# Routing of an attention and experts kernel: early places ahead of the last logits, row and column by an integer mask, ScalarE squares the decay and marks four tiles

## The reference

```python
# 1. decaying linear attention: B=2, H=8, S=768, D=64, blocks of 64
intra = (q_b @ k_b^T * Dmask) @ v_b                  # Dmask = lam ** (i - j) for i >= j
inter = (q_b * lam ** (i + 1)) @ kv_state
out_b = intra + inter
kv_state = lam ** 64 * kv_state + (k_b * lam ** (63 - j))^T @ v_b
# 2. mixture of experts: N=1536 tokens, 512 features, E=8 experts of width 1024, the best one only
logits = x @ w_gate; e = argmax(logits); gate = softmax(logits)[e]
y = gate * (relu(x @ w1[e]) @ w2[e])
# 3. dense layer, width 2048
h = y @ w_in; out = (h - tanh(h)) @ w_out
```

## Time and profile before

| | us |
|---|---|
| median of 3 runs | 526.89 |
| lowest, highest | 526.42, 528.42 |
| profiled execution, its own time | 527.13 |
| its span, first to last instruction | 525.4 |
| TensorE busy in the span | 507.6 |
| VectorE, ScalarE, GpSimd busy | 361.3, 258.2, 318.1 |
| mean granted TensorE clock | 0.993 |

### The profile page before, as it was taken

The page is one execution under the profiler, slowest core; times in us unless marked ns, Lnnn a source line. Parts: engine busy times, 40 slices in busy tenths (PEclk is TensorE's granted clock), DMA queues, the critical chain, the costliest instruction groups (busy, mean ns, idle before and its releaser), DMA issues.

```text
span 525.4 us, 10760 instructions
## 1 busy us (share of the span) xinstructions
PE 507.6 (97%) x3809; PEld 450.0 (86%) x3810; DVE 361.3 (69%) x546; ACT 258.2 (49%) x474; POOL 318.1 (61%) x261
## 2 busy tenths in 40 slices
PE   5999989999999999999999999999999999999994
PEld 4878879999999999999888888888888888888883
DVE  7555546654545545454599999979987766997781
ACT  1333417666666666656454545544444444544441
POOL 4857057655545545555499898958765454865543
PEclk9999899999999999999999999999999999999998
DMA  8879348778777777774620000001100000100002
GB/s 310 305 250 361 146 120 284 240 198 233 211 222 236 197 232 230 203 238 120 218 106 1 1 2 0 1 0 40 41 1 1 0 1 3 58 21 2 1 0 80
DMA packets 32409, 64.54 MB, mean 123 GB/s; under 512 B 3696, under 2 KB 7792, under 8 KB 32368
## 3 DMA queue, kind: packets, MB, share of 16 engines
q1 hardware_dynamic: 30448, 57.71, 34.8%
q0 software_dynamic: 1920, 6.29, 3.5%
HBM read 57.69 MB, written 6.29 MB: 122 GB/s over the span
## 4 chain that ended last, share of the span: by engine, by line
PE 92%; DMA 3%; POOL 1%; DVE 1%; issue 1%; ACT 1%; SPq 0%; ACTq 0%; POOLq 0%; DVEq 0%
PE bank L325 27%; PE bank L327 27%; PE bank L326 27%; PE bank L1177 3%; PE bank L1151 2%; DMA x_sorted<-token_rows,tokid 2%; PE bank L1197 1%; DMA qk_in<-in_qk_t_dram 1%; PE bank L1163 1%; PE bank L1188 1%; PE bank L1204 1%; POOL x_sorted L634 1%; POOL w_l L626 0%; PE bank L1362 0%; PE bank L1267 0%
## 5 line engine op out<-in xcount | busy, mean ns | idle before, releaser
L626 POOL TENSOR_TENSOR w_l<-wst,w_h 128x512 fp32r<-128x512 f32 x64 | 87.0, 1359 | 78.0 <-ACT w_h L737 77.9
L675 POOL TENSOR_SCALAR big<-h_sq 128x512 uint8<-128x512 f32 x48 | 80.4, 1674 | 36.0 <-ACT h_sq L823 35.8
L689 POOL TENSOR_TENSOR g_l<-g,g_h 128x512 fp32r<-128x512 f32 x46 | 61.2, 1331 | 43.0 <-ACT g_h L833 43.0
L325 PE MATMUL bank<-wo_h,g_h 128*128 128x512 f32 x192 | 75.5, 393 | 0.1
L327 PE MATMUL bank<-wo_l,g_h 128*128 128x512 f32 x192 | 75.1, 391 | 0.0
L326 PE MATMUL bank<-wo_h,g_l 128*128 128x512 f32 x192 | 74.6, 389 | 0.0
L327 PE MATMUL bank<-x_l,win_h 128*128 128x512 f32 x188 | 74.3, 395 | 0.0
L325 PE MATMUL bank<-x_h,win_h 128*128 128x512 f32 x188 | 73.9, 393 | 0.0
L326 PE MATMUL bank<-x_h,win_l 128*128 128x512 f32 x188 | 73.7, 392 | 0.0
L325 PE MATMUL bank<-xs_h,w_h 128*128 (+1 forms) x256 | 70.8, 276 | 0.8 <-DVE xs_l L1045 0.8
L325 PE MATMUL bank<-h_h,w_h 128*128 128x232 f32 x256 | 70.3, 275 | 0.0
(11 more groups left out here) (152 smaller groups left out, 1102.8 us busy)
## 6 DMA issues: line engine op xcount, KB each, us to landing
wst<-in_w_dram SPq DMA_DIRECT2D x128, 256.0 KB, 3.0
qk_in<-in_qk_t_dram SPq DMA_DIRECT2D x12, 512.0 KB, 6.4
kv_in<-in_kv_dram SPq DMA_DIRECT2D x12, 512.0 KB, 5.6
win<-in_w_in_dram SPq DMA_DIRECT2D x8, 512.0 KB, 4.6
wo<-in_w_out_dram SPq DMA_DIRECT2D x8, 512.0 KB, 8.4
token_rows<-x_sb SPq DMA_DIRECT2D x12, 256.0 KB, 5.9
x_sorted<-token_rows,tokid POOLq DMA_INDIRECT x12, 4.2
out_dram<-rows,tokid POOLq DMA_INDIRECT x12, 3.0
```

Source lines behind the costliest of these rows:

```text
L325: pe.matmul(dst, lh, rh, start=start, stop=False, skip_group_check=True)
L626: pool.tensor_tensor(w2_l[:, j % STG], wst2[:, j % STG], w2_h[:, j % 2].bitcast(F32), ALU.subtract).then_inc(w2l_ready, 1)
L675: pool.tensor_scalar(big[:, f % 2], h_sq[:, f % 2], T * T, None, ALU.is_ge).then_inc(big_ready, 1)
L689: pool.tensor_tensor(g_l[:, f % 2], g[:, f % 2], g_h[:, f % 2].bitcast(F32), ALU.subtract).then_inc(gl_ready, 1)
```

## The change

- SyncE loads both forms of the decay factors in one DMA. ScalarE squares them (six squares) and makes `q_pow` by doubling, with four multiplies a step; VectorE's squares and GpSimd's doubling go.
- GpSimd's half of the mask waits until VectorE has finished the first half with its diagonal (`mask_ready` 1).
- TensorE runs the first four heads of tile 0 on v ahead of the scores of tile 1, and waits for `w_gate` at the first gate logits only.
- Behind the loop: places of tiles 0 to 7, then the last gate logits, then both last transposes, then the places of tiles 8 to 11. Before: transposes of tile 10, last logits, transposes of tile 11, early places, three keep-awakes, late places.
- Column and row of a place come from an integer mask (place and -128, and the rest); the comparison with 13 limits and its reduction go.
- ScalarE marks the rows of tiles 8 to 11, as relu(1 - (row - n)^2), between its last x_sb and its first expert weights; VectorE marks tiles 0 to 7.
- GpSimd runs one small indirect DMA of 16 rows (from w_out, into a buffer that is written later) once all tiles have their outputs, and waits for it, ahead of its wait for the token numbers.

The diff without declarations of buffers and semaphores, the DMA of the factors and some unchanged lines:

```diff
@@ -563,6 +566,7 @@
 
             pool.wait_ge(far_step, 6)
             pool.wait_ge(near_step, 10)
+            pool.wait_ge(mask_ready, 1)
             mask_blocks(pool, head_halves[1]).then_inc(late_blocks_ready, 1)
 
...
@@ -588,21 +592,13 @@
 
             pool.wait_ge(mask_ready, 2)
             k_decayed(0)
-            pool.wait_ge(lam_pair_in, 16)
-            pool.tensor_copy(q_pow[:, :, 0:1], lam_pair_sb[:].rearrange("p (a n) -> p a n", n=1)).then_inc(qpow_step, 1)
-            n = 1
-            while n < P:
-                pool.wait_ge(qpow_step, n.bit_length())
-                pool.tensor_tensor(q_pow[:, :, n:2 * n], q_pow[:, :, 0:n],
-                                   q_pow[:, :, n - 1:n].to_broadcast([P, PAIRS, n]), ALU.mult).then_inc(qpow_step, 1)
-                n *= 2
             k_decayed(1)
-            pool.wait_ge(qpow_step, POW_STEPS)
 
             pool.memset(ones[:], 1.0).then_inc(consts, 1)
             pool.wait_ge(consts, 2)
             pool.affine_select(out=tri[:], in_=ones[:], compare_op=ALU.is_gt, fill=0.0, base=0,
                                pattern=[[1, P]], channel_multiplier=-1).then_inc(consts, 1)
+            pool.wait_ge(qpow_step, POW_STEPS)
             for t in range(B, NT):
                 q_decayed(t)
                 if t < NT - B:
...
+            pool.memset(some_row[:], 0).then_inc(consts, 1)
+            pool.wait_ge(consts, 10)
+            pool.wait_ge(o_done, NT)
+            pool.indirect_dma_start(
+                out=x_sorted[0:REHEARSED, NT - 1, :], out_offset=None, in_=w_out,
+                in_offset=bass.IndirectOffsetOnAxis(ap=some_row[0:REHEARSED, :], axis=0)).then_inc(rehearsed, 16)
+            pool.wait_ge(rehearsed, 16)
             for u in range(UN):
                 pool.wait_ge(x_stored[u], 16 * (NT // UN))
...
         def _(act):
 
+            act.wait_ge(lam_in, 16)
+            for i in range(1, 7):
+                ge(act, lam_step, i - 1)
+                act.activation(lam_pow[:, i], lam_sb[:, 0:H] if i == 1 else lam_pow[:, i - 1],
+                               ACT.Square).then_inc(lam_step, 1)
+
+            act.copy(q_pow[:, :, 0:1], lam_sb[:, H:].rearrange("p (a n) -> p a n", n=1)).then_inc(qpow_step, 1)
+            n = 1
+            while n < P:
+                act.wait_ge(qpow_step, n.bit_length())
+                for p in range(PAIRS):
+                    i = act.mul(q_pow[:, p, n:2 * n], q_pow[:, p, 0:n], q_pow[:, p, n - 1:n])
+                i.then_inc(qpow_step, 1)
+                n *= 2
+
             def x_t(t):
...
+
+            act.wait_ge(consts, 9)
+            act.wait_ge(row_ready, 1)
+            for t in range(BY_DVE, NT):
+                act.activation(off_row[:, t], row_no[:], ACT.Square, bias=row[:, t:t + 1],
+                               scale=-1.0).then_inc(off_row_ready, 1)
+            for t in range(BY_DVE, NT):
+                act.wait_ge(off_row_ready, t - BY_DVE + 1)
+                act.activation(in_row[:, t], off_row[:, t], ACT.Relu, bias=1.0, scale=-1.0).then_inc(late_rows_ready, 1)
 
             w1_high(0, 0)
...
@@ -872,13 +899,7 @@
             dve.tensor_copy(diagonal[:], own_block[:]).then_inc(seeds, 1)
 
             dve.wait_ge(lam_in, 16)
-            dve.tensor_tensor(lam_pow[:, 1], lam_sb[:], lam_sb[:], ALU.mult).then_inc(lam_step, 1)
             dve.wait_ge(seeds, 5)
-
-            def square(i):
-
-                dve.wait_ge(lam_step, i - 1)
-                dve.tensor_tensor(lam_pow[:, i], lam_pow[:, i - 1], lam_pow[:, i - 1], ALU.mult).then_inc(lam_step, 1)
 
...
@@ -887,11 +908,9 @@
                 if i:
                     dve.wait_ge(lam_step, i)
                     dve.wait_ge(near_step, 2 * i)
-                lam_n = lam_sb[:] if i == 0 else lam_pow[:, i]
+                lam_n = lam_sb[:, 0:H] if i == 0 else lam_pow[:, i]
                 dve.tensor_tensor(near_part[:, :, n:end], near[:, :, 0:end - n], every(lam_n, end - n),
                                   ALU.mult).then_inc(near_step, 1)
-                if i + 2 < 7:
-                    square(i + 2)
                 dve.wait_ge(near_step, 2 * i + 1)
                 dve.tensor_tensor(near[:, :, n:end], near[:, :, n:end], near_part[:, :, n:end], ALU.add).then_inc(near_step, 1)
...
@@ -989,16 +1008,15 @@
             dve.wait_ge(places_done, 1)
             dve.tensor_tensor(place_of[:], psPos, one_hot[:], ALU.mult).then_inc(route_step, 1)
             dve.wait_ge(route_step, 3)
-            dve.tensor_reduce(place_f[:], place_of[:], AX.X, ALU.add).then_inc(route_step, 1)
+            with nc.allow_low_precision(reason="whole numbers below 4096"):
+                dve.tensor_reduce(place_i[:], place_of[:], AX.X, ALU.add).then_inc(route_step, 1)
             dve.wait_ge(route_step, 4)
-            dve.tensor_tensor(past_col[:], col0[:, :].rearrange("p (a e) -> p a e", a=1).to_broadcast([P, NT, NT + 1]),
-                              place_f[:, :].rearrange("p (t a) -> p t a", a=1).to_broadcast([P, NT, NT + 1]),
-                              ALU.is_le).then_inc(route_step, 1)
+            dve.tensor_scalar(col[:], place_i[:], -P, None, ALU.bitwise_and).then_inc(route_step, 1)
             dve.wait_ge(route_step, 5)
-            dve.tensor_reduce(col[:], past_col[:, :, 1:], AX.X, ALU.add).then_inc(route_step, 1)
-            dve.wait_ge(route_step, 6)
-            dve.scalar_tensor_tensor(row[:], col[:], -float(P), place_f[:], ALU.mult, ALU.add).then_inc(row_ready, 1)
-            dve.tensor_tensor(in_col[:], past_col[:, :, 0:NT], past_col[:, :, 1:], ALU.subtract).then_inc(route_step, 1)
+            dve.tensor_tensor(row[:], place_i[:], col[:], ALU.subtract).then_inc(row_ready, 1)
+            dve.tensor_tensor(in_col[:], col0[:, :].rearrange("p (a e) -> p a e", a=1).to_broadcast([P, NT, NT]),
+                              col[:, :].rearrange("p (t a) -> p t a", a=1).to_broadcast([P, NT, NT]),
+                              ALU.is_equal).then_inc(route_step, 1)
             dve.wait_ge(row_ready, 1)
...
@@ -1010,10 +1028,10 @@
                     ALU.is_equal).then_inc(rows_ready, t1 - t0)
 
             mark_rows(0, 4)
-            dve.wait_ge(route_step, 7)
+            dve.wait_ge(route_step, 6)
             dve.tensor_tensor(ids[:, :, 0], in_col[:], tile_no[:], ALU.mult)
             dve.tensor_scalar(ids[:, :, 1], in_col[:], token_no[:, 0:1], None, ALU.mult).then_inc(ids_ready, 1)
-            for t in range(4, NT, 4):
+            for t in range(4, BY_DVE, 4):
                 mark_rows(t, t + 4)
...
@@ -1172,6 +1190,7 @@
                 for h in range(H):
                     a, p = divmod(h, PAIRS)
                     if t == 0 and h == PAIRS:
+                        scores(1)
                         pe.wait_ge(sm_ready, 1)
                     g, half = divmod(p, 2)
...
@@ -1206,9 +1227,7 @@
                 j.then_inc(logits_done, 1)
 
             scores(0)
-            scores(1)
             pe.wait_ge(ident_ready, 1)
-            pe.wait_ge(w_gate_in, 16)
             for t in range(NT):
                 if t > 1:
...
@@ -1221,12 +1240,6 @@
                     gate_logits(t - 1)
                 if t < NT - B:
                     state_step(t)
-            x_transposes(NT - 2)
-            gate_logits(NT - 1)
-            x_transposes(NT - 1)
-            pe.wait_ge(consts, 3)
...
@@ -1241,8 +1254,11 @@
                                   start=False, stop=True, skip_group_check=True)
                 return i
 
+            pe.wait_ge(consts, 3)
             places(0, EARLY, 0)
-            keep_awake(pe, 3)
+            gate_logits(NT - 1)
+            x_transposes(NT - 2)
+            x_transposes(NT - 1)
             places(EARLY, NT, 1).then_inc(places_done, 1)
             for t in range(NT):
                 i = pe.matmul(psCnt, ones[:], one_hot_b[:, t], start=t == 0, stop=t == NT - 1)
...
@@ -1252,7 +1268,10 @@
             keep_awake(pe, 8)
             pe.wait_ge(ids_ready, 1)
             for t in range(NT):
-                pe.wait_ge(rows_ready, t + 1)
+                if t < BY_DVE:
+                    pe.wait_ge(rows_ready, t + 1)
+                else:
+                    pe.wait_ge(late_rows_ready, t - BY_DVE + 1)
                 for v in range(2):
                     i = pe.matmul(psId, in_row[:, t], ids[:, t, v], start=t == 0 and v == 0, stop=t == NT - 1 and v == 1)
...
```

More of the change, by code:

```diff
@@ L31, with decay_attention_moe_kernel @@
 POLY = (-0.019268172807322046, 2.644734663353291, -0.07151553627681556, 6.536064820179784)
-def decay_attention_moe_kernel(nc, qk_t, kv, lam_all, lam_pair, w_gate, w1, w2, w_in, w_out, out):
+def decay_attention_moe_kernel(nc, qk_t, kv, lam_both, w_gate, w1, w2, w_in, w_out, out):
     B, H, D = 2, 8, 64
@@ L63, in decay_attention_moe_kernel @@
     GATE_LAG = 3
+    BY_DVE = 8
+    REHEARSED = 16
     EARLY = NT - 4
@@ L242, in decay_attention_moe_kernel @@
         rows_ready = sem("rows_ready")
+        off_row_ready = sem("off_row_ready")
```

(3 more changed lines are left out.)

23 lines of the change are left out of this document (12 added, 11 removed).

## The result

| | before | after |
|---|---|---|
| median of 5 runs each | 526.84 | 523.81 |
| lowest, highest | 526.42, 528.42 | 523.43, 524.97 |
| profiled execution, its own time | 527.13 | 523.49 |
| its span | 525.4 | 521.7 |
| mean granted TensorE clock | 0.993 | 0.997 |

What follows compares the result with a forecast made beforehand. TensorE, busy 507.6 of 525.4 us, was taken as the bound. Terms +0.1 - 1.84 - 0.54 + 0.45 - 0.5 = -2.33 took 527.1 to 524.8, stated as 524.7; 8 in 10 range 523.4 to 526.6.

Steps and rivals of the forecast that it cites:

- Start: Kernel start up to the first heads: TensorE's work the same and contiguous in either order, +0.1 us, bounds -0.4 and +0.5.
- far ready: Start: GpSimd's far chain, fed by ScalarE's squares, ready near 5.8 us; it ended at 6.81 before.
- Order at the end of the attention: Behind the attention loop: reordered places and transposes, three keep-awakes gone, place_of starting at 62.05 instead of 63.88; -1.84 us.
- Clock: Routing: a later low-clock stretch could slow the eight keep-awakes and delay tokid to 66.8; half booked, +0.45 us.
- Places to token numbers: From place_of to tokid: 3.8 us instead of 4.34, by integer mask and ScalarE's marks; -0.54 us.
- Column and row: Behind place_of: one bitwise and replaces comparison and reduction, so the first in_row starts 0.49 us earlier.
- The marks by ScalarE: Rows of the last four tiles: squares and relus at a 0.3 us pitch, done 3.5 us after place_of starts.
- Rehearsal: First gather: removing first-use cost saves up to 0.8 us, capped by TensorE's pace; -0.5 us, bounds 0 and -0.6.
- Rival (c): First gather: its 0.92 us gap is recurring semaphore and address work, rehearsal does nothing; -1.9, 525.2; chance 0.47 together with forecast.
- Stores: Stores of x before the gathers: landed by 65 us, before tokid, at no cost.
- rival (a): Routing: clock does not fall or falls harmlessly, and gathers start all 0.8 us earlier; -3.2, 523.9; chance 0.33.
- The signs that I had listed: Start and routing in the profile after: expected times for first heads, q_pow, place_of, tokid, first gather and first product (73.5).

Runs made afterwards that it cites:

- run 9: Changed kernel with the whole old start (squares on VectorE, q_pow on GpSimd, old mask and head order), single factor DMA kept: 524.93, ratio 0.9958.
- run 2: Changed kernel with the old order of first heads, mask halves and w_gate wait, ScalarE's squares and q_pow kept: 523.0, ratio 0.9923.
- run 11: The kernel of run 2 timed again beside the changed kernel: 523.30, ratio 0.9938.
- run 3: Changed kernel with the old order behind the attention loop, including the three keep-awakes: 524.82, ratio 0.9977.
- run 5: The kernel before, unchanged, profiled once more: 527.63 (one run).
- run 10: Changed kernel without the eight keep-awakes behind the last places: 529.42 (one run).
- run 8: Changed kernel with column and row found by comparison and reduction as before, ScalarE's marks kept: 524.76, ratio 0.9952.
- run 4: Changed kernel with VectorE marking the rows of all twelve tiles, ScalarE none: 523.89, ratio 0.9951.
- run 1: Changed kernel without the rehearsal DMA: 523.99, ratio 0.9953.
- run 6: Changed kernel with VectorE's first two low parts of weights held until the first gather landed: 524.42, ratio 0.9948.
- run 7: Changed kernel with the rehearsal started once place rows are known, its landing awaited only before tile 11's gather: 524.65, ratio 0.9945.
- run 12: Changed kernel, unchanged, profiled and timed again: 524.61, ratio 0.9963.

## Why the prediction was right, and where not

**Start, booked +0.1, measured +0.13.** Right in size and right in the steps: first heads at 8.53 (booked 8.4), mask half 0.69 (0.65), far ready near 5.9 (5.8), q_pow done at 10.50 (11.5). What it did not see is that two of the change's parts cancel. Squares on ScalarE with the old order bring the scores of tile 2 to 12.79 and 12.02, against 13.36 of the kernel before and 13.59 of run 9, because they end the wait for s_m of run 9. Some of that is the moment at which TensorE's pace changes (see the last section), which differs between executions. The state's first update starts ahead of it in nearly every trace: at 11.79 and 11.46 in runs 2 and 11, 12.36 to 12.60 in the kernel before and run 9, 12.49 in the changed kernel. So the squares give 0.6 to 1.1 us. The new head order takes it back: TensorE stands 1.39 us ahead of 8.53 for a mask which, in the old order, would have been made under scores(1). I had argued "the work is the same, and it is contiguous in either order"; it is contiguous behind the first heads, but those start later than scores(1) could. When scores(1) can start is set by a landing, at 7.61 to 8.32 us in the five traces with the old order, so the gain varies too.

**Order at the end of the attention, booked -1.84.** This is the term that failed in its working. In the first pair of profiles it seems met (63.88 - 58.68 = 5.20 against 3.21, less the 0.12 us that the last logits slipped: -1.87). But I had taken the three keep-awakes at 1.41 us, a price at the lower clock level. At the higher level they take 0.90, the first places less than the 0.9 booked, and the order is worth 0.7 to 0.8 (runs 3 and 5). The other 1.16 are those of a clock that had fallen.

**Clock, booked +0.45.** It went the other way: in no profile of the changed kernel, nor of its variants but run 10, did the clock fall in the routing. How often it falls can be estimated from the mean granted clock of each run. 3.4 us at 0.51 take 0.0032 off the mean of a span of 525. Every profiled run also has the lower level in the last 1.8 to 4.4 us of its span, which takes 0.002 to 0.004; so a mean of 0.995 or less speaks for a fall elsewhere, but does not prove it. Of the kernel before, 27 of 74 runs have such a mean, with a median of 527.99, and the other 47 have 526.20. Of the changed kernel and its timed variants together it is 6 of 101; set by set 3 of 38 against 10 of 29, 0 of 30 against 12 of 24, and 3 of 28 against 5 of 21, besides the first 5 runs with none. So something that these kernels share makes the fall rarer. For the changed kernel alone, 2 of 17 runs, and 2 of 12 against 5 of 21 in its own set, that is not shown. Why the clock falls in some executions of one program and not in others no run here tells. Run 3 keeps the old order and had 2 such runs of 12, so the order by itself doesn't explain the difference.

**Places to token numbers, booked -0.54, measured -0.89** (4.34 us in both profiles of the kernel before, 3.45 and 3.46 after). Column and row took -0.49 as worked out (run 8). The marks by ScalarE took -0.41 more (run 4), where I had booked next to nothing: the four squares came at a pitch of 0.30 as booked (1.28 us for four), but the relus, whose bias is a constant and not a pointer, at 0.2 (0.89 for four), so the late rows were done at S + 3.13, with S the start of place_of, instead of S + 3.5. That was my lower bound for the pitch. The Trainium skill ("ScalarE: Activation LUTs", ACT is a hardware spline evaluator) says that a pointer operand adds about 93 ns to one with immediates, and that neighbours overlap by about as much; the two pitches here, 0.30 and 0.20, agree.

**Rehearsal, booked -0.5, measured -0.17 at the second turn and nothing at the first product.** Rival (c) is nearly what happened. Of the 0.8 us that I had put down to first use, 0.18 was (run 1); 0.09 was VectorE beside it (run 6). The gap stays: 0.83 to 0.86 us with a rehearsal 7 us before, and 0.91 behind a store's landing with one 7 us or 1.7 us before (runs 6 and 7). The first two scatters at the end, also indirect DMAs from GpSimd, start 0.28 us behind their releaser; what the gather's gap is made of was not found. The Trainium skill ("GPSIMD Engine Reference", 2.1 Instruction dispatch) has about 6 us for the first call of a freshly loaded kernel. Run 1 has no earlier indirect DMA, and its first gather lost 0.18 us. No run here shows a load of 6 us; whether there was one to make, or whether it hid in the engine's 14.28 us of idle time, the traces don't tell.

**Stores, booked at nothing, since "they land by 65, before tokid".** They do land by 65 in most traces, at 64.11 in the changed kernel. But tokid's end is now at 64.33 instead of the 66 that I had in mind, so the two are 0.22 us apart, and 0.05 in run 12. In runs 6, 7 and 10 the last store landed 0.33, 0.14 and 0.27 us behind tokid's end (at 64.69, 66.04 and 64.62), and the gather started 0.91 us behind that landing: the gap behind tokid was 1.25, 1.06 and 1.18 us instead of 0.84, 0.2 to 0.4 us of cost. It is the next bound of this path: a further gain between place_of and tokid would be met there.

**The sum.** At full clock the terms that traces support are +0.13 - 0.72 - 0.89 = -1.5, inside the interval of the measured gain. That gain is -2.1 over all runs; among runs with a mean clock over 0.995 the medians are 526.20 and 523.97, so -2.2, with an interval of -2.8 to -1.1 from resampling both sets (526.29 and 524.31, -2.0, in the one set that has both kernels). So 0.6 or 0.7 us of it have no term, and since the gain is no smaller where the clock did not fall, the rarer fall doesn't supply them.

The first pair of profiles differs by 3.64 us. The parts along its path: +0.13 at the start; -1.44 for one iteration of the attention loop, which took 5.67 us instead of 4.23, 1.01 of it the stand of the earlier trace rows, which no part of the change reaches; -1.87 from the logits of tile 10 to place_of, of which 1.16 are the clock; -0.89 to tokid; and +0.4 behind the first product, 0.24 of it by longer waits for gathers. Such stands ("issue", 0.1 to 1.0 us, near 28.0, 34, 46.5 or 53.5 us) came and went in variants and in the kernel before alike: 0.39 in its second profile, 0.95 and 0.29 in run 7, none in runs 1, 3, 8, 10, 11, 12.

So the time was right in part by luck. An order priced at the wrong clock (1.1 too much) and a rehearsal (0.3 to 0.5 too much) stood against a loss by the clock that didn't come (0.45), marks sized too small (0.35) and the 0.6 to 0.7 without a term. The signs that I had listed show it. The first heads (8.53), q_pow (10.50) and place_of to the first in_row (1.09) came as said. But place_of came at 60.71 instead of 62.0, tokid at 64.16 instead of 65.9 to 66.8, the gather 0.84 us behind it instead of within 0.3, and the first product at 71.90 instead of 73.5. Of rival (a) the half on the clock came true, the half on the gathers didn't. No single undoing costs over 0.4 us in its median against 524.57 (runs 3, 8, 9; runs 1 and 4 are below it); with 10 or 12 runs each and a scatter of 3 us they can't be told from one another, and the shares rest on the traces.

## What to carry to other kernels

Before pricing a keep-awake or any short matmul from one profile, look at the granted clock of that very stretch, and at the mean clock of the other runs: a price taken at the lower level is not there to win in most executions. When an engine is given its input earlier, ask what it could have been doing meanwhile: here an order that starts the newly early work first wasted what had made it early. A gap behind a wait is first use only if a rehearsal closes it. A lead at one milestone is worth following to the end: here 1.5 us were gone some 20 us later, in waits for later gathers.

## What the runs showed of the hardware

- VectorE and GpSimd at work on 128x512 float32 at once: the one that began first kept its time, the other lost. GpSimd first by 0.02 or 0.03 us (kernel before, run 9): its mask product took 1.05 us, as alone, and VectorE's 1.57 instead of 0.69. VectorE first by 0.11 (run 2): its product took 0.69, GpSimd's 1.49, and VectorE's predicated copy behind it 1.46 instead of 0.73.
- The same 16 scores matmuls take 2.08 us early and 1.16 from tile 3 on, at a granted clock of 1.00 in both, so the granted clock doesn't tell of this pace. It changed at 11.3 us in run 11, 12.6 in run 4, about 13.8 in the changed kernel and 14.4 in run 12; what changed it was not found.
- The fall of the clock is not a property of the program alone: one kernel showed a mean of 0.995 or less in 27 of 74 runs, and those were 1.8 us slower in the median. The one traced fall cost 1.16 us up to place_of.
- The first gather starts 0.83 to 0.92 us behind whatever releases it last, be it VectorE's token numbers or the landing of a store (runs 1, 6, 7, 10 and after); a second rehearsed call doesn't change that.
- A store of 256 KB landed 3.6 us behind the start of its issue (run 6), though the DMA engines there show a share of 0.62 from 62 to 63 us, 0.06 in the next and 0.01 in the one after: most of the data had moved 1.7 us before the landing at 64.69.
